# The head of a fused three-stage kernel: first chunks, norm sums, the first tile's operands and the score scaling rearranged

## The reference

```
qn = q / (norm over tokens(q) + 1e-6);  kn likewise
s  = kn^T @ qn / tau                     # 256 x 256
a  = softmax(s, last axis, + 1e-9)
x  = v @ a                               # 6016 x 256
h  = x @ w_in                            # 256 -> 2048
g  = h if h >= 1, 0 if h <= -1, else (h + 1)^2 / 4
y  = g @ w_out                           # 2048 -> 256
xn = y / rms(y) * rms_g
out = (silu(xn @ w_gate) * (xn @ w_val)) @ w_out2   # 256 -> 1536 -> 256
```

## Time and profile before

| | us |
|---|---|
| median of three runs | 1099.82 |
| lowest, highest | 1098.47, 1099.93 |
| profiled execution, its time | 1098.53 |
| profiled execution, its span | 1096.70 |

### The profile page before, as it was taken

How to read it: one execution, slowest core, us unless ns; L and a number is a source line. 1 busy time by engine, 2 the same in 40 slices (tenths; PEclk the granted TensorE clock), 3 DMA queues, 4 the chain that set the end, 5 groups by cost and what they waited for, 6 DMA issues and landing times.

```text
span 1096.7 us, 14355 instructions
## 1 busy us (share of the span) xinstructions
PE 1086.5 (99%) x4970; PEld 908.5 (83%) x4970; DVE 869.7 (79%) x1271; ACT 800.6 (73%) x1149; POOL 2.3 (0%) x13
## 2 busy tenths in 40 slices
PE   8999999999999999999999999999999999999998
PEld 7877888888888888888888888888888888888998
DVE  5878888887887887889999888787877878777665
ACT  5678898898898898897887666567567556556554
POOL 0000000000000000000000000000000000000000
PEclk9999999999999999999999999999999999999999
DMA  9910112002002000003222010111111002011012
GB/s 341 315 25 1 22 37 58 1 20 58 1 20 53 1 20 20 1 30 106 58 92 58 1 39 20 20 37 39 37 20 39 11 10 53 1 20 20 1 20 54
DMA packets 109018, 48.77 MB, mean 44 GB/s; under 512 B 85266, under 2 KB 99218, under 8 KB 108946
## 3 DMA queue, kind: packets, MB, share of 16 engines
q1 hardware_dynamic: 108946, 47.86, 15.8%
HBM read 35.52 MB, written 12.32 MB: 44 GB/s over the span
## 4 chain that ended last, share of the span: by engine, by line
PE 95%; DVE 2%; ACT 1%; DMA 1%; issue 1%; SPq 0%; DVEq 0%; ACTq 0%
PE ps L1224 17%; PE ps L1226 17%; PE ps L1225 17%; PE ps L1242 8%; PE ps L1244 8%; PE ps L1243 8%; PE ps L1264 5%; PE ps L1263 5%; PE ps L1265 5%; PE ps L1299 3%; PE ps L1284 1%; PE ps L1288 1%; PE ps L1286 1%; PE ps L1194 1%; DMA qk_sb<-in_k_dram 1%
## 5 line engine op out<-in xcount | busy, mean ns | idle before, releaser
L430 ACT ACTIVATE s<-ps 128x512 f32<-128x512 f32 (+1 forms) x360 | 210.2, 588 | 35.5 <-PE ps L1226 21.5
L1224 PE MATMUL ps<-xc_hi,wc_hi 128*128 128x512 f32 (+1 forms) x504 | 195.6, 388 | 0.1
L1225 PE MATMUL ps<-xc_lo,wc_hi 128*128 128x512 f32 (+1 forms) x504 | 194.3, 386 | 0.0
L1226 PE MATMUL ps<-xc_hi,wc_lo 128*128 128x512 f32 (+1 forms) x504 | 194.3, 385 | 0.0
L1242 PE MATMUL ps<-g_hi,wo_hi 128*128 128x512 f32 (+1 forms) x384 | 150.2, 391 | 0.4 <-DVE g_lo L804 0.2
L430 ACT ACTIVATE h_hi<-cg 128x512 fp32r<-128x512 f32 (+1 forms) x144 | 88.3, 619 | 83.1 <-DVE cg L902 80.1
L1243 PE MATMUL ps<-g_lo,wo_hi 128*128 128x512 f32 (+1 forms) x384 | 148.1, 386 | 0.0
L1244 PE MATMUL ps<-g_hi,wo_lo 128*128 128x512 f32 (+1 forms) x384 | 148.0, 386 | 0.0
L788 DVE TENSOR_TENSOR h_sb<-ps,s 128x512 f32<-128x512 f32 (+1 forms) x144 | 97.8, 679 | 59.0 <-PE ps L1226 58.3
L804 DVE TENSOR_TENSOR g_lo<-h_sb,g_hi 128x1024 fp32r<-128x1024 f32 (+1 forms) x96 | 114.9, 1197 | 10.3 <-ACT g_hi L430 9.3
L882 DVE TENSOR_TENSOR h_lo<-cg,h_hi 128x512 fp32r<-128x512 f32 (+1 forms) x144 | 97.5, 677 | 30.1 <-ACT h_hi L430 26.4
(11 more groups left out here) (130 smaller groups left out, 1859.6 us busy)
## 6 DMA issues: line engine op xcount, KB each, us to landing
qk_sb<-in_q_dram SPq DMA_DIRECT2D x10, 512.0 KB, 10.2
qk_sb<-in_k_dram SPq DMA_DIRECT2D x10, 512.0 KB, 10.5
y_scratch<-y_sb SPq DMA_DIRECT2D x10, 512.0 KB, 3.0
xraw<-y_scratch SPq DMA_DIRECT2D x10, 512.0 KB, 4.3
out_dram<-outT_sb SPq DMA_DIRECT2D x80, 64.0 KB, 1.9
vstage<-in_v_dram SPq DMA_DIRECT2D x64, 64.0 KB, 2.4
wo_raw<-in_moe_w_out_dram SPq DMA_DIRECT2D x7, 512.0 KB, 9.5
w_in_raw<-in_moe_w_in_dram SPq DMA_DIRECT2D x4, 512.0 KB, 12.1
```

What stands on the lines that cost most here:

```text
L430: return nc.scalar.activation(dst, src, ACT.Copy, **kw)
L1224: nc.tensor.matmul(dst, w_h, x_h, start=p in ("p1", "p2", "p7"), stop=False, skip_group_check=True)
L1225: nc.tensor.matmul(dst, w_h, x_l, start=False, stop=False, skip_group_check=True)
L1226: nc.tensor.matmul(dst, w_l, x_h, start=False, stop=True, skip_group_check=True).then_inc(made[p], 1)
```

## The change

- The chunk list starts with 1, 1, 2, 2, 2 in place of 1, 1, 2; there is one chunk of four less, so 17 chunks in place of 15.
- v's first tile is loaded after all of q and k, transposed on PE after all scores, and copied out of PSUM by DVE, behind the two maxima, in place of ACT during the scores. `make_w1(0)` then waits for it.
- The norm matmuls come after chunk NC-3, the qrow matmuls after chunk NC-2, both ahead of the last scores.
- ACT copies the row of q norms to SBUF, and one DVE instruction for each half scales and multiplies the scores. `scaled` is gone.
- ACT, not DVE, copies the transposed e.
- All `xc_sum`, `xc_high`, `xc_low` of tile 0 stand among the w1 steps and inside group 0. `wo1_high(0)` moves on ACT behind `w1_copy(7)`, `wo1_low(0)` on DVE behind `w1_low(3)`, ahead of c22 of group 0.
- The three `keep_warm` calls behind the scores (2, 6 and 3 matmuls) are gone.

The diff, without the declarations of tiles and semaphores:

```diff
@@ -41,7 +41,7 @@
     RB = 4
-    RCH = [1, 1, 2] + [RB] * ((NB - 5) // RB) + [2, 1]
+    RCH = [1, 1, 2, 2, 2] + [RB] * ((NB - 11) // RB) + [2, 1]
     RAT = [sum(RCH[:i]) for i in range(len(RCH))]
@@ -354,8 +353,7 @@
                                  allow_slow_non_contiguous=True).then_inc(small_loaded, 16)
-                if c == 6:
-                    sp.dma_start(v0_raw[:], v[0, 0:WIDE, :].rearrange("(b p) c -> p b c", p=P)).then_inc(v0_loaded, 16)
+            sp.dma_start(v0_raw[:], v[0, 0:WIDE, :].rearrange("(b p) c -> p b c", p=P)).then_inc(v0_loaded, 16)
             for c in range(FC):
@@ -455,7 +453,10 @@
                 n, slot = half(X % WT), PRODUCTS[p][1]
-                act.wait_ge(xsum_ready, 4 * X + (1 if p in ("p1", "p2") else 4))
+                if X == 0 and p in ("p1", "p2"):
+                    act.wait_ge(v0_copied, 1 if p == "p1" else 2)
+                else:
+                    act.wait_ge(xsum_ready, 4 * X + (1 if p in ("p1", "p2") else 3 if X == 0 and p == "p7" else 4))
                 if p in ("p1", "p2") and 1 <= X <= WT:
@@ -558,32 +559,27 @@
                                      ACT.Square).then_inc(squared, 1)
-                if c == 8:
-                    act.wait_ge(v0_filled, 1)
-                    for h in range(2):
-                        copy(xraw[:, 2 * h:2 * h + 2, :],
-                             ps[:, V0_BANK + 2 * h:V0_BANK + 2 * h + 2, :]).then_inc(v0_copied, 1)
-                if c >= 10:
-                    for p in {10: ORDER[0:3], 11: ORDER[3:5], 12: ORDER[5:7]}.get(c, []):
-                        xc_high(0, p)
             act.wait_ge(norms_summed, 1)
...
             nc.scalar.activation(unread[:, 1:2], ones[:, 0:1], ACT.Exp)
-            act.wait_ge(scale_ready, 1)
-            act.wait_ge(scored, NC)
-            for a in range(CT):
-                copy(scaled[:, a, :], ps[:, a, 0:C], scale=k_scale[:, a:a + 1]).then_inc(scaled_ready, 1)
+            act.wait_ge(qrow_filled, 1)
+            copy(qrow[:], ps[:, QROW_BANK, 0:C]).then_inc(qrow_ready, 1)
             for a in range(CT):
...
                                      accum_out=e_sum[:, a:a + 1]).then_inc(exp_ready, 1)
-            wo1_high(0)
+            act.wait_ge(eT_filled, 1)
+            copy(eT_sb[:], ps[:, ET_BANK, :].rearrange("p (a i) -> p a i", a=CT)).then_inc(eT_ready, 1)
+            xc_high(0, "p1")
+            xc_high(0, "p2")
             act.wait_ge(sum_ready, 1)
...
             w1_high(0, 1)
+            xc_high(0, "p7")
             w1_copy(2)
+            xc_high(0, "p6")
             w1_high(1)
@@ -595,6 +591,8 @@
                     square(n1 - 1, 1)
+                else:
+                    xc_high(0, "p4")
                 spare(s7, "p7", c22_ready, n1, n, 3, s7_ready)
@@ -611,12 +609,15 @@
                     if p == 0:
+                        xc_high(0, "p5")
+                        xc_high(0, "p3")
                         w1_high(2)
...
                         w1_copy(7)
+                        wo1_high(0)
                     elif p in (1, 3):
@@ -931,11 +932,6 @@
                                             ALU.add).then_inc(added, 1)
-                if c in (8, 9):
-                    for i in ((0, 1) if c == 8 else (2, 3)):
-                        xc_sum(0, i)
-                for p in {10: ORDER[0:2], 11: ORDER[2:3]}.get(c, []):
-                    xc_low(0, p)
             base = adds_until(NC - 1)
@@ -943,8 +939,6 @@
                                     ALU.add).then_inc(added, 1)
-            for p in ORDER[3:5]:
-                xc_low(0, p)
             steps = [0]
@@ -960,26 +954,34 @@
             last.then_inc(diag_ready, 1)
-            nc.vector.tensor_scalar(k_scale, inv_norms[:, CT:2 * CT], inv_tau, None, ALU.mult).then_inc(scale_ready, 1)
-            dve.wait_ge(qrow_filled, 1)
+            step(nc.vector.tensor_scalar(k_scale, inv_norms[:, CT:2 * CT], inv_tau, None, ALU.mult))
+            dve.wait_ge(qrow_ready, 1)
+            dve.wait_ge(scored, NC)
             for a in range(CT):
-                dve.wait_ge(scaled_ready, a + 1)
-                step(nc.vector.tensor_tensor(scores[:, a, :], ps[:, QROW_BANK, 0:C], scaled[:, a, :], ALU.mult))
+                step(nc.vector.scalar_tensor_tensor(scores[:, a, :], ps[:, a, 0:C], k_scale[:, a:a + 1], qrow[:],
+                                                    ALU.mult, ALU.mult))
                 nc.vector.tensor_reduce(neg_max[:, a:a + 1], scores[:, a, :], axis=AX_X, op=ALU.max,
                                         negate=True).then_inc(max_ready, 1)
+            for a in range(CT):
+                dve.wait_ge(v0_filled, a + 1)
+                nc.vector.tensor_copy(xraw[:, 2 * a:2 * a + 2, :],
+                                      ps[:, V0_BANK + 2 * a:V0_BANK + 2 * a + 2, :]).then_inc(v0_copied, 1)
             dve.wait_ge(exp_ready, CT)
...
             nc.vector.reciprocal(inv_sum, e_sum1).then_inc(sum_ready, 1)
-            dve.wait_ge(eT_filled, 1)
-            nc.vector.tensor_copy(eT_sb[:], ps[:, ET_BANK, :].rearrange("p (a i) -> p a i", a=CT)).then_inc(eT_ready, 1)
-            for p in ORDER[5:7]:
-                xc_low(0, p)
+            xc_low(0, "p1")
+            xc_low(0, "p2")
+            xc_sum(0, 0)
             w1_sums(0)
             w1_low(0, 0)
+            xc_sum(0, 1)
+            xc_sum(0, 2)
             w1_low(0, 1)
+            xc_low(0, "p7")
+            xc_sum(0, 3)
+            xc_low(0, "p6")
             w1_sums(1)
             w1_low(1)
-            wo1_low(0)
@@ -987,6 +989,8 @@
                 combine(h[:, 0, 0:n], s1, s1_ready, "p2", n1, n, 2, c11_ready)
+                if n1 == 0:
+                    xc_low(0, "p4")
                 if into:
@@ -1001,10 +1005,13 @@
                 if n1 == 0:
+                    xc_low(0, "p5")
                     w1_sums(2)
+                    xc_low(0, "p3")
                     w1_sums(3)
...
                     w1_low(3)
+                    wo1_low(0)
                 if T == WT - 2 and p == 1:
@@ -1299,42 +1306,40 @@
                 last.then_inc(scored, 1)
-                if c == 7:
-                    pe.wait_ge(v0_loaded, 16)
-                    pe.wait_ge(const_ready, 1)
-                    for a in range(CT):
-                        for b in range(2 * NCH):
-                            bank = V0_BANK + 2 * a + b // NCH
-                            last = nc.tensor.transpose(ps[:, bank, (b % NCH) * P:(b % NCH + 1) * P],
-                                                       v0_raw[:, b, a * P:(a + 1) * P], ident[:])
-                    last.then_inc(v0_filled, 1)
                 if c == 8:
...
                                      stop=True).then_inc(tau_filled, 1)
-            pe.wait_ge(added, adds_until(NC - 1) + 2)
-            for i in range(2):
-                for a in range(CT):
-                    last = nc.tensor.matmul(ps[:, NORM_BANK, CT * i + a:CT * i + a + 1],
-                                            sumsq[:, i, 0, a * P:(a + 1) * P], ones[:, 0:1],
-                                            start=i == 0 and a == 0, stop=True, skip_group_check=True)
-            last.then_inc(norms_summed, 1)
-            pe.wait_ge(v0_copied, 2)
-            keep_warm(2)
-            pe.wait_ge(diag_ready, 1)
+                if c == NC - 3:
+                    pe.wait_ge(added, adds_until(NC - 1) + 2)
+                    for i in range(2):
+                        for a in range(CT):
+                            last = nc.tensor.matmul(ps[:, NORM_BANK, CT * i + a:CT * i + a + 1],
+                                                    sumsq[:, i, 0, a * P:(a + 1) * P], ones[:, 0:1],
+                                                    start=i == 0 and a == 0, stop=True, skip_group_check=True)
+                    last.then_inc(norms_summed, 1)
+                if c == NC - 2:
+                    pe.wait_ge(diag_ready, 1)
+                    for a in range(CT):
+                        last = nc.tensor.matmul(ps[:, QROW_BANK, a * P:(a + 1) * P], ones[:], diag[:, a, :],
+                                                start=True, stop=True)
+                    last.then_inc(qrow_filled, 1)
+            pe.wait_ge(v0_loaded, 16)
+            pe.wait_ge(const_ready, 1)
             for a in range(CT):
-                last = nc.tensor.matmul(ps[:, QROW_BANK, a * P:(a + 1) * P], ones[:], diag[:, a, :], start=True,
-                                        stop=True)
-            last.then_inc(qrow_filled, 1)
-            keep_warm(6)
+                for b in range(2 * NCH):
+                    bank = V0_BANK + 2 * a + b // NCH
+                    last = nc.tensor.transpose(ps[:, bank, (b % NCH) * P:(b % NCH + 1) * P],
+                                               v0_raw[:, b, a * P:(a + 1) * P], ident[:])
+                last.then_inc(v0_filled, 1)
             for a in range(CT):
...
             last.then_inc(eT_filled, 1)
-            keep_warm(3)
```

(8 more changed lines are left out.)

## The result

| | before | after |
|---|---|---|
| median of five runs, us | 1099.82 (1098.47 to 1100.53) | 1105.67 (1104.96 to 1107.27) |
| ratio after to before, 95% interval | | 1.0057 (1.0042 to 1.0072) |
| profiled execution, us | 1098.53 | 1105.67 |
| its span | 1096.70 | 1103.90 |
| mean granted TensorE clock | 1.000 | 0.995 |

The change makes the kernel slower by 0.57%, about 6.3 us (5.85 between the two medians). Three slips in the text above first, on which nothing in the sum hung. The new list has 16 chunks (5 + 9 + 2), not 17, so it issues two more DMAs, not four. In the first 50 us of the kernel before the DMAs move 352 GB/s, 17.6 of the 48.77 MB, so not most of it. And what the trace shows of a float32 matmul is two records (`keep_warm(6)` leaves 12); it does not show in how many passes the array works.

What follows compares the result with a forecast made beforehand. TensorE, busy 99%, bounds the kernel, so only the startup can change: 8.55 us lost after make_w1(0) less 3.5 gained before it gives +5.05, 1103.6; with half the run level 1104.2, range 1101.0 to 1107.0 and 0.3 more.

Steps and rivals of the forecast that it cites:

- signs of being wrong: PE waits under 7 us between first w1 matmul and second stage, or a later stretch giving time back.
- Score end: End of the score stage in the startup: forecast at 49.2 us in place of 50.17.
- make_w1(0): First w1 matmul after the softmax: starts at 53.25, not 56.73, waiting for v's copy; front gains 3.5 us.
- Wait for s1: PE waits before p6 in group 0 until ACT copies s1, behind w1_high(1): 2.6 us.
- Second and third wait: Group 0: PE waits 1.1 us before p4 for xc_low p4, then 0.95 before p5 for its xc parts.
- Wait for c22: PE waits before p3 in group 0 for c22, behind wo1_high(0) and wo1_low(0): 4.4 us, the largest.
- From combine22 to the second stage: Order as in the old kernel, so piece1(0,0) starts 5.12 us after combine22.
- rival C: PE's clock runs slow behind the 4.4 us wait, so p3, p1, p2, p7 take double: +2.1, 1106.3; chance 0.13.
- The level: Unprofiled runs before had a median 1.29 us above the profiled one; half of that was added to the forecast.
- Rival A: Moved xc work fills idle DVE and ACT time, only the front's 3.5 us gain shows: 1095.7; chance 0.11.
- Rival D: Landing of q and k bounds the score end, which stays near 50.2; loss +6.05, 1105.2; chance 0.05.
- B: It levels out within 2 us: the four group 0 waits sum to about 4.5; +1.0, 1100.2; chance 0.11.

Runs made afterwards that it cites:

- warm_gaps: The changed kernel with useless matmuls filling PE's two long waits of group 0, 9 before p6 and 13 before p3; ratio 1.0044 to the kernel before, span 1102.1.
- reorder: wo_early with w1_high(1) moved behind group 0's s2 copy on ACT, w1_sums(1) and w1_low(1) later on DVE; ratio 0.9999 to the kernel before, span 1097.3.
- both_fronts: Kernel before with the change's front edits, v's first tile loaded last, and xc work laid in waits; median 1096.25, ratio 0.9971 to the kernel before, span 1094.7.
- wo_early: The changed kernel with wo1_high(0) moved behind xc_high p2 on ACT and wo1_low(0) behind combine21 on DVE; ratio 1.0028 to the kernel before, span 1100.1.

## Why the prediction was right, and what it missed

The direction, the place and the two long waits held; the time, 1105.67, lies in the range and 1.5 us above the forecast of 1104.2. One term of the loss, the slower clock, stood at nothing in the forecast. One of the prediction's own signs of being wrong came true: it named under 7 us of PE waits between the first w1 matmul and the second stage, and they sum to 6.82. With the clock held up (warm_gaps) that stretch takes 85.69 - 53.60 = 32.09 us, 8.74 more than before against the forecast 8.55; at the real clock it is 10.26 more, partly as longer records in place of waits. So the chains of work were read rightly, and the sum of the waits was not. Point by point:

- **Score end.** Forecast 49.2, measured 49.20. The wait for the landing at 13.4 came as said; norms and qrow found everything ready. That it fits to the hundredth is luck: the chunks gave 0.58 us (27.49 for 28.07) and not 0.72, and the norm and qrow matmuls took 0.79 and 0.44, not 1.0 and 0.5.
- **make_w1(0).** Forecast 53.25, measured 53.47. `scalar_tensor_tensor` of 256 columns took 0.48, not 0.42, so the second maximum ended at S+1.91, not S+1.71; the two copies of v took 1.22 each as assumed and ended at 53.38. The trace names ACT's copy of e as releaser, but that ended at 52.87; v's copy is the later of the two conditions. That it alone holds PE there was not tried. Gain of the front 3.26, forecast 3.5.
- **Wait for s1.** Forecast 2.6, measured 2.85. By `reorder` it is the order that makes it: w1_high(1) ahead of s1 on ACT, fed by w1_sums(1) on DVE.
- **Second and third wait.** Forecast 1.1 and 0.95. In the profile they are hardly there, because p6 and the make_w1 records ran at 1.2 GHz and filled them; with the clock up (warm_gaps) they are 0.88 and 0.88.
- **Wait for c22.** Forecast 4.4, measured 3.83. PE was through make_w1(7) at 78.14 in place of the forecast 79.8 - 3.5 = 76.3, and p3 started at 81.97 in place of 80.7, so PE was 1.8 us late and p3 1.3. With the clock up PE is through at 77.14 and p3 starts at 81.31, 4.2 later. combine22 was forecast, on the real clock, at 83.5 - 3.5 = 80.0; measured 81.14, and 80.57 with the clock up.
- **From combine22 to the second stage.** Taken from the old trace as 5.12; measured 87.08 - 81.14 = 5.94, since the nine records of p3, p1 and p2 took 0.39 to 0.50 us each in the chain; those of p7 took 0.23 again.
- **The sum.** +5.05 on the span, measured +7.2. With the clock held up (warm_gaps) +5.4. So the term that was mis-sized is the clock: I left it out of the forecast and gave it 13% as rival C. C had the mechanism. Its price of +2.1 was for the fall behind the long wait, and that one cost 0.8 (5.94 for 5.12); the fall behind the 2.85 us wait, which C did not have, cost the other 0.6 (combine22 at 81.14 for 80.57). That C's 1106.3 lies nearer to the result than the forecast is therefore partly luck.
- **The level.** The half level of 0.65 us made up for part of the clock that was left out. On the span the forecast missed by 2.15 us, on the time by 1.5.
- **Rival A**, that late work fills idle time, fell for this order of instructions. `reorder` shows that it isn't the amount: with all of that work still late the loss is gone. And its other part, that the 3.5 us of the front would show, still did not come true there; the front's gain went into the waits of 0.90 and 1.75 us and, in the profiled execution, into slow records at 54 to 58 us. `both_fronts` gets 2.0 of the 3.5.
- **Rival D** fell (score end 49.20), **B** too (its four waits sum to about 4.5; measured 6.82, and the clock adds to them).

## What to carry to other kernels

When work moves from a place where it was hidden to a startup with several engines in strict order, string out each engine's order by measured durations and look for what stands ahead of the next instruction that frees the bound engine; 2.3 us of work ahead of c22 cost 3.4, the clock included. Edits that look independent can need each other: the finer chunks and the early norms gained nothing that the timing could tell while v's load and its work stood in mid-scores. And price a new long wait of TensorE twice, once as a wait and once for the slower records behind it.

## What the runs showed of the hardware that I had not expected

- A wait of 2.85 us of PE had the granted clock at 0.52 in the five microseconds behind it in the changed kernel, and one of 2.81 had 0.50 in wo_early. A wait of 1.39 in wo_early and one of 1.75 in reorder had 1.00 behind them. Filled with useless matmuls, the waits for s1 and c22 left it at 1.00.
- The two levels in the runs of the kernel before, which I could only split in half in the prediction, go with the clock. In 48 runs beside the experiments, the 12 with a mean clock of 0.998 took 1099.88 to 1100.96 us; of the other 36 all but one (1100.22) took 1097.32 to 1099.42. So in the kernel before, too, the mean clock is lower in a quarter of the executions, and these are about 2 us longer; where it falls was not profiled. In the eight runs of both_fronts, whose warm-up calls behind the scores stay, it was 0.999 or more.
